# The first chunk of an RWKV, soft-MoE and FFN kernel: products with u moved between engines, and one load of expert weights asked for earlier

## Chip, core and metric

One core of one Trainium2 chip. The metric is the device time of one execution in microseconds (us); lower is better. A run of the kernel before is told by the median of three timed executions; one more execution was profiled.

## What is computed

Three stages in a row, all in fp32 at the interface. The first, an RWKV recurrence, is the one that the change touches:

```python
def _attn_ref(r, k, v, w, u):           # r, k, v: (4, 8, 768, 48); w, u: (8, 48)
    for t in range(S):
        kt, vt, rt = (k[:, :, t], v[:, :, t], r[:, :, t])
        cur = np.einsum('bhd,bhe->bhde', u[None] * kt, vt)
        y[:, :, t] = np.einsum('bhd,bhde->bhe', rt, state + cur)
        state = w[None, :, :, None] * state + np.einsum('bhd,bhe->bhde', kt, vt)
```

Its output, laid out as x of 3072 tokens by 384, goes through a soft mixture of 8 experts with 4 slots each: logits = x @ phi, a softmax over the tokens that gathers the slots' inputs, per expert relu(slot @ w1) @ w2, and a softmax over the slots that spreads the results. The last stage is h = x @ w_in (384 by 2048), g = h * sigmoid(1.702 h), g @ w_out.

## The kernel before

The recurrence is done in chunks of 128 time steps: 6 chunks (C) of 4 batches (B), so 24 steps (c, b), which this text numbers n = 4c + b, from batch 0 to batch 23. The work of one batch:

- VectorE scales r and k, which come as one transposed tile rkb, with powers of w (`scale`, L761, writes rks); TensorE multiplies them to scores (`scores`, L369); VectorE masks the scores (`mask`, L783, writes at).
- The term of the own time step, the bonus sum(r * k * u) * v. The product r*k is made by GpSimd from a second, untransposed tile krb (`bonus`, L1189, writes rkn), the product with u (ubc, u on all 128 partitions) by GpSimd, but in the first chunk by VectorE (L777). VectorE sums over the 48 channels of a head (`bonus_sum`, L770, writes dds). GpSimd multiplies v with the sums (`bonus_values`, L1209, writes vd). TensorE turns vd into the outputs' accumulators (`bonus_turns`, L388, line L396), in the first chunk one batch late, except for the chunk's last batch.
- TensorE adds the earlier state's part (`earlier`, L402) and scores times v (`outputs`, L419), ScalarE copies the result to yt (`columns`, L996).
- GpSimd makes scaled keys (`scaled_keys`, L1201, writes kk, with wkn, powers of w that TensorE turned and ScalarE copied), TensorE multiplies them with v (`state`, L430), VectorE adds that to the state (`new_state`, L798), which ScalarE first decays with four activations (`decay`, L1006).
- TensorE turns yt back (`tokens`, L441), ScalarE copies it (`rows`, L1014). From the second chunk on, the soft-MoE's running softmax over tokens runs with it.

Every engine runs its own program in the order of the code and waits on semaphores. TensorE's order for a batch is: earlier part of the batch before, scores of this batch, bonus turns (first chunk), outputs, state and token turns of batches before. The functions `step` of each engine set this order. The first chunk is written out, chunks 1 to 4 are a loop, the last chunk is written out.

SyncE (SP) issues the loads in one line: rkb, krb and v of a batch, with two buffers for rkb and krb. The load of rkb n waits until VectorE has scaled batch n-2, that of krb n until GpSimd has made the keys of n-2; each waits in the line, so what is behind it waits too. Behind each batch's loads from the second chunk on stand one or two pieces (512 KB each) of the expert weights w1 (`load_w1`, L283), 24 in all, four of them in the last chunk. ScalarE's queue loads the identity, u (128 copies), the mask, and, after it has copied wkn, phi in five small loads (L992, L994). At the start TensorE does dummy products (`keep_warm`, L361) until the first scores are possible: ten, and seven more after the first scores.

After the scan come the experts (L556 to L615) and the FFN (`tile`, L696), in which TensorE works through three fp32r products per 128x512 tile.

## Time and profile before

| | us |
|---|---|
| median of three timed executions | 389.01 |
| lowest and highest | 386.53, 389.36 |
| the profiled execution | 385.76 |
| its span in the trace | 383.8 |

The span runs from the first to the last recorded instruction; the profiled execution's own time is 1.96 us longer. A "batch" in the scan is a period of some 4.4 us. The times in all rows are counted from the span's start. In a row of the timeline the first number is the start, the second the time until the merged instructions have ended, and in brackets stands how long the engine was idle before and what ended that. fp32 products are issued in two passes, so that a row of eight products counts x16.

### The profile page before, as it was taken

To read this page: it belongs to the slowest core of one execution; us is meant where nothing else is said; L and a number is where in the kernel's file an instruction comes from. 1 tells how busy PE (TensorE), PEld (TensorE's weight loads), DVE (VectorE), ACT (ScalarE), POOL (GpSimd) and SP (SyncE) were. 2 spreads that over 40 slices of the span, in tenths; PEclk is the share of its full clock that TensorE was granted. 3 is DMA by queue.
4 is the path that set the end of the run, shared out by engine and by line. 5 is a ranking of instruction groups with operands and counts; after the bars stand their busy time and mean duration, and the time that the engine had idled before them with its cause. 6 is when DMAs were issued, how large, how long until landed. Compare 5 with 4: busy or idle time off the path is not lost.

```text
span 383.8 us, 9102 instructions
## 1 busy us (share of the span) xinstructions
PE 370.8 (97%) x3212; PEld 291.3 (76%) x3212; DVE 236.2 (62%) x433; ACT 189.4 (49%) x410; POOL 92.4 (24%) x109
## 2 busy tenths in 40 slices
PE   5699999999999999999999999999999999999996
PEld 5578787878877344568888888888888888888885
DVE  6988696978784201678756556555555555555550
ACT  1345454544435341676564456445644564465552
POOL 4777897888672100000000000000000000000000
PEclk9999999999999999999999999999999999999999
DMA  7899999999999899600011002000200020002002
GB/s 232 293 340 392 395 360 401 376 404 400 402 345 412 344 379 413 258 0 2 1 40 45 0 2 82 0 0 0 82 0 0 0 82 0 0 0 82 0 2 82
DMA packets 21797, 63.76 MB, mean 166 GB/s; under 512 B 3088, under 2 KB 6816, under 8 KB 21392
## 3 DMA queue, kind: packets, MB, share of 16 engines
q1 hardware_dynamic: 20864, 63.09, 43.3%
q10 hardware_dynamic: 912, 0.39, 0.6%
q8 instruction: 14, 0.23, 0.2%
q14 instruction: 7, 0.06, 0.0%
HBM read 58.75 MB, written 4.72 MB: 165 GB/s over the span
## 4 chain that ended last, share of the span: by engine, by line
PE 91%; DVE 3%; DMA 2%; issue 1%; ACT 1%; POOL 1%; SPq 0%; DVEq 0%; ACTq 0%
PE bank L639 11%; PE bank L637 11%; PE bank L638 11%; PE bank L377 6%; PE pair L425 6%; PE pair L637 6%; PE pair L638 5%; PE pair L639 5%; PE bank L622 4%; PE pair L413 3%; PE pair L396 3%; PE bank L584 3%; PE bank L446 3%; PE bank L564 2%; PE bank L437 2%; DMA vb<-v 2%
## 5 line engine op out<-in xcount | busy, mean ns | idle before, releaser
L921 DVE TENSOR_TENSOR gf<-bank,sg 128x512 f32<-128x512 f32 x72 | 49.7, 691 | 59.3 <-ACT sg L1119 58.9
L1119 ACT ACTIVATE sg<-bank 128x512 f32<-128x512 f32 x72 | 42.9, 598 | 73.4 <-PE bank L622 73.4
L637 PE MATMUL bank<-glo,whi 128*128 128x512 f32 x190 | 73.9, 389 | 0.0
L639 PE MATMUL bank<-ghi,wlo 128*128 128x512 f32 x190 | 73.9, 389 | 0.0
L638 PE MATMUL bank<-ghi,whi 128*128 128x512 f32 x190 | 73.9, 389 | 0.0
L927 DVE TENSOR_TENSOR glo<-gf,ghi 128x512 fp32r<-128x512 f32 x96 | 66.2, 690 | 1.0 <-ACT ghi L1125 0.7
L1125 ACT ACTIVATE ghi<-gf 128x512 fp32r<-128x512 f32 x96 | 60.0, 625 | 2.0 <-DVE gf L921 1.9
L639 PEld LDWEIGHTS bank<-ghi,wlo 128*128 128x128 f32 x190 | 35.7, 188 | 7.4
L637 PEld LDWEIGHTS bank<-glo,whi 128*128 128x128 f32 x190 | 35.7, 188 | 7.4
L638 PEld LDWEIGHTS bank<-ghi,whi 128*128 128x128 f32 x190 | 35.7, 188 | 7.4
L767 DVE TENSOR_TENSOR rks<-rkb,bank 112x512 f32<-112x512 f32 x48 | 30.7, 681 | 12.9 <-PE pair L413 6.6
L637 PE MATMUL pair<-glo,whi 128*128 128x512 f32 x95 | 37.2, 391 | 0.5 <-DVE glo L927 0.4
L638 PE MATMUL pair<-ghi,whi 128*128 128x512 f32 x95 | 37.0, 389 | 0.0
L639 PE MATMUL pair<-ghi,wlo 128*128 128x512 f32 x95 | 37.0, 389 | 0.0
L793 DVE COPY_PREDICATED at<-keep,bank 128x512 f32<-128x512 int32 x48 | 32.6, 731 | 1.3 <-PE bank L377 0.9
L377 PE MATMUL bank<-rks 48*128 48x128 f32 x384 | 27.9, 284 | 5.2 <-DVE rks L767 3.8
L377 PEld LDWEIGHTS bank<-rks 48*128 48x128 f32 x384 | 23.4, 187 | 9.5 <-issue 7.9
L921 DVE TENSOR_TENSOR gf<-pair,sg 128x512 f32<-128x512 f32 x24 | 16.6, 691 | 22.6 <-ACT sg L1119 22.5
L1002 ACT ACTIVATE yt<-pair 112x512 f32<-112x512 f32 x24 | 14.3, 597 | 29.3 <-PE pair L425 29.3
L622 PE MATMUL bank<-ct,mst 128*128 (+1 forms) x72 | 27.9, 392 | 0.4 <-DVE mst L951 0.4
L1194 POOL TENSOR_TENSOR rkn<-krb 128x384 f32<-128x384 f32 x24 | 24.1, 1003 | 12.1 <-DMA krb<-kr 11.7
L425 PE MATMUL pair<-at,vb 128*48 128x128 f32 x384 | 25.9, 277 | 0.0
(183 smaller groups left out, 512.6 us busy)
## 6 DMA issues: line engine op xcount, KB each, us to landing
ring<-w SPq DMA_DIRECT2D x24, 512.0 KB, 6.3
rkb<-rk SPq DMA_DIRECT2D x23, 512.0 KB, 6.0
krb<-kr SPq DMA_DIRECT2D x24, 384.0 KB, 5.7
ring<-w SPq DMA_DIRECT2D x4, 1536.0 KB, 13.8
ring<-w SPq DMA_DIRECT2D x8, 768.0 KB, 9.7
vb<-v SPq DMA_DIRECT2D x24, 192.0 KB, 5.6
out<-ob SPq DMA_DIRECT2D x18, 256.0 KB, 2.1
ring<-win SPq DMA_DIRECT2D x3, 1024.0 KB, 14.9
```

The lines of the kernel that those rows point to most:

```text
L377: last = pe.matmul(SC[i][:, hp * CH:(hp + 1) * CH], rks[s, b % 2, 1, hp, :], rks[s, b % 2, 0, hp, :], start=True, stop=True)
L425: last = pe.matmul(YT[i][o0:o0 + D, a * CH:(a + 1) * CH], vb[:, b, 2 * (a + 2 * w) + i, :], at[:, b % 2, i, a + 2 * w, :], start=False, st ...
L622: pe.matmul(HB[f % 4][:, :], mst[:, f * P:(f + 1) * P], ct_flat[:, bass.ds(i * TT, TT)], start=True, stop=True).then_inc(hh_ps, 1)
L637: pe.matmul(o, w_hi, lo, start=(f == 0), stop=False)
L638: pe.matmul(o, w_hi, hi, start=False, stop=False)
L639: pe.matmul(o, w_lo, hi, start=False, stop=(f == KF - 1)).then_inc(prod_ps, 1)
L767: dve.tensor_tensor(rks[a, b % 2, x, :, :], rkb[a, b % 2, x, :, :], w[a, :, :], ALU.mult)\
L793: dve.copy_predicated(at[:, b % 2, half, :, :], keep[:, :].unsqueeze(1).to_broadcast([P, 4, CH]), SC[half][:, :].rearrange("p (h t) -> p h ...
L921: dve.tensor_tensor(gf[:, f % 2, :], bank[f % 4][:, :], sg[:, f % 2, :], ALU.mult).then_inc(gf_ok, 1)
L927: dve.tensor_tensor(glo[:, f % 4, :], gf[:, f % 2, :], ghi[:, f % 4, :], ALU.subtract)\
L1119: act.activation(sg[:, f % 2, :], bank[f % 4][:, :], ACT.Sigmoid, scale=1.702).then_inc(sg_ok, 1)
L1125: act.activation(ghi[:, f % 4, :], gf[:, f % 2, :], ACT.Copy).then_inc(ghi_ok, 1)
```

## The change

It touches the first chunk (c = 0) and three orders.

- u is loaded to one partition; DVE sets 128 ones in a row of lnat, TensorE multiplies ones and u (a product over one row, 384 columns), ScalarE copies the result to all partitions of ubc. The dummy products are three ahead of it, six behind it (WARM) and eight after the first scores.
- In the first chunk GpSimd does the products with u, as in the others. Its `step` is split: the r*k product of batch 1 stands ahead of the scaled keys of batch 0.
- In the first chunk ScalarE makes vd from v, by eight activations of 48 columns with the sum as scale, one per head, ahead of `columns` of the batch before. It no longer decays the zero states of batches 0 to 2.
- VectorE scales batch n+1 ahead of mask of batch n for all n of the first chunk, and sums batch n between the two. The sum waits for the bonus turns of two batches back, no longer for vd alone.
- phi's five loads move from ScalarE's queue to SP, ahead of batch 2's loads.
- One piece of w1 is asked for behind batch 3's loads; every later piece moves up by one, and the last batch has none.

```diff
@@ -40,7 +40,7 @@
 LEAD = 3
-WARM = 10
+WARM = 6
@@ -190,6 +190,7 @@
             sem(n) for n in ("lt_ps", "l_ok", "cm_ok", "nm_ok", "ex_ok", "al_ok", "tr_ps", "tr_ok", "p_ps", "run_ok"))
+        s_u, ones_ok, u_ps, u_ok, vd_first = (sem(n) for n in ("s_u", "ones_ok", "u_ps", "u_ok", "vd_first"))
         nm_new, l_new, mask_go, tiles_go = (sem(n) for n in ("nm_new", "l_new", "mask_go", "tiles_go"))
@@ -297,16 +298,22 @@
             load_v(0, 1)
+            for o0, w in HEADS:
+                for p0, i in HEADS:
+                    sp.dma_start(phs[o0:o0 + D, :, :].rearrange("p (a i) s -> p a i s", i=2)[:, :, i, :],
+                                 phi[p0:p0 + D, 2 * w:2 * w + 2, :]).then_inc(s_phi, 16)
+            sp.dma_start(phs[D:64, :, :], phi[D:64, :, :]).then_inc(s_phi, 16)
             step(0, 2, 0, 0)
-            step(0, 3, 0, 0)
+            step(0, 3, 0, 1)
             for dst, src in ((same[:, :], match), (jcol[:, :], jsel), (pick[:, :, :], sel)):
...
                 for b in range(B):
-                    step(c, b, (B + 1) * (c - 1) + b, 1 if b < B - 1 else 2)
+                    step(c, b, (B + 1) * (c - 1) + 1 + b, 1 if b < B - 1 else 2)
             for b in range(B):
-                step(C - 1, b, (B + 1) * (C - 2) + b, 1)
+                step(C - 1, b, (B + 1) * (C - 2) + 1 + b, 1 if b < B - 1 else 0)
@@ -363,6 +370,12 @@
+            keep_warm(LG, 3)
+            pe.wait_ge(ones_ok, 1)
+            pe.wait_ge(s_u, 16)
+            pe.matmul(YN[:, 0:DM], lnat_flat[0:1, 0:P], ubc[0:1, :, :].rearrange("p h e -> p (h e)"),
+                      start=True, stop=True).then_inc(u_ps, 1)
             keep_warm(LG, WARM)
@@ -380,17 +393,18 @@
                     pe.wait_ge(wks_done, 1)
+                    pe.wait_ge(u_ok, 1)
                     for i in range(HP):
...
                     last.then_inc(wkn_ps, 1)
-                    keep_warm(LG, 7)
+                    keep_warm(LG, 8)
...
                 wait(pe, yt_ok, n)
-                wait(pe, vd_ok, n + 1)
+                wait(pe, *((vd_first, n + 1) if is_first(c) else (vd_ok, n - B + 1)))
                 for i in range(2):
@@ -721,6 +735,7 @@
+            dve.memset(lnat_flat[0:1, 0:P], 1.0).then_inc(ones_ok, 1)
             dve.memset(acc[:, :], 0.0).then_inc(run_ok, 1)
@@ -769,22 +784,15 @@
                 n = B * c + b
-                if is_first(c):
-                    dve.wait_ge(rk_ok, n + 1)
-                    if b == 0:
-                        dve.wait_ge(s_const, 16 * 2)
-                    dve.tensor_tensor(rkn[:, b % 2, :, :], rkn[:, b % 2, :, :], ubc[:, :, :], ALU.mult)\
-                       .then_inc(rku_ok, 1)
                 dve.wait_ge(rku_ok, n + 1)
-                wait(dve, vd_ok, n - 1)
+                wait(dve, vd_used, n - 1)
                 dve.tensor_reduce(dds[:, b % 2, :], rkn[:, b % 2, :, :], AX_X, ALU.add).then_inc(dd_ok, 1)
...
                     dve.wait_ge(zeroed, 5)
-                    dve.wait_ge(s_const, 16 * 2)
+                    dve.wait_ge(s_const, 16)
                 for half in range(2):
@@ -798,7 +806,11 @@
                 dve.wait_ge(st_ps, n + 1)
-                dve.wait_ge(sdec, HP * (n + 1))
+                if is_first(c):
+                    dve.wait_ge(s_new, 1)
+                else:
+                    dve.wait_ge(sdec, HP * (n - B + 2))
                 dve.tensor_tensor(st[a, b, :, :].rearrange("p h e -> p (h e)"),
@@ -843,16 +855,14 @@
                     slot_max(c - 1)
+                if more:
+                    scale(*following(c, b))
                 if is_first(c) and b:
-                    mask(c, b)
-                    scale(*following(c, b))
-                else:
-                    if more:
-                        scale(*following(c, b))
-                    mask(c, b)
+                    bonus_sum(c, b)
+                mask(c, b)
                 if is_last(c) and b == 2:
                     row_sum(*early)
-                if more:
+                if more and (tail or b == B - 1):
                     bonus_sum(*following(c, b))
@@ -979,19 +989,28 @@
             act.dma_start(idt[:, :], ident).then_inc(s_ident, 16)
-            for dst, src in ((ubc[:, :, :].rearrange("p h e -> p (h e)"), u.partition_broadcast(P)),
-                             (keep[:, :], strict)):
-                act.dma_start(dst, src).then_inc(s_const, 16)
+            act.dma_start(ubc[0:1, :, :].rearrange("p h e -> p (h e)"), u.partition_broadcast(1)).then_inc(s_u, 16)
+            act.dma_start(keep[:, :], strict).then_inc(s_const, 16)
+            act.wait_ge(u_ps, 1)
+            act.activation(ubc[:, :, :].rearrange("p h e -> p (h e)"), YN[:, 0:DM], ACT.Copy).then_inc(u_ok, 1)
...
                            ACT.Copy).then_inc(wkn_ok, 1)
-            for o0, w in HEADS:
-                for p0, i in HEADS:
-                    act.dma_start(phs[o0:o0 + D, :, :].rearrange("p (a i) s -> p a i s", i=2)[:, :, i, :],
-                                  phi[p0:p0 + D, 2 * w:2 * w + 2, :]).then_inc(s_phi, 16)
-            act.dma_start(phs[D:64, :, :], phi[D:64, :, :]).then_inc(s_phi, 16)
+            def bonus_values(c, b):
+                n = B * c + b
+                act.wait_ge(dd_ok, n + 1)
+                act.wait_ge(v_in[b], 16)
+                wait(act, vd_used, n - 1)
+                if b == 0:
+                    act.wait_ge(zeroed, 5)
+                for w in range(2):
+                    for x in range(HP):
+                        h = HP * w + x
+                        last = act.activation(vd[:, b % 2, x, w, 0:D], vb[:, b, h, :], ACT.Copy,
+                                              scale=dds[:, b % 2, h:h + 1])
+                last.then_inc(vd_first, 1)
@@ -1042,12 +1061,14 @@
                 tail = not is_first(c)
+                if not tail:
+                    bonus_values(c, b)
                 if tail and b == 1:
...
                 if not is_first(c, b):
-                    if not is_last(prev(c, b)[0]):
+                    if not is_first(prev(c, b)[0]) and not is_last(prev(c, b)[0]):
                         decay(*prev(c, b))
@@ -1186,16 +1207,20 @@
-            def bonus(c, b):
+            def products(c, b):
                 n = B * c + b
...
                     .then_inc(rk_ok, 1)
-                if is_first(c):
-                    return
+            def factors(c, b):
+                n = B * c + b
+                s = b % 2
                 pool.wait_ge(rk_ok, n + 1)
+                if is_first(c, b):
+                    pool.wait_ge(u_ok, 1)
                 pool.tensor_tensor(rkn[:, s, :, :], rkn[:, s, :, :], ubc[:, :, :], ALU.mult).then_inc(rku_ok, 1)
@@ -1211,8 +1236,6 @@
                 wait(pool, vd_used, n - 1)
-                if is_first(c, b):
-                    pool.wait_ge(zeroed, 5)
                 pool.tensor_tensor(vd[:, b % 2, :, :, 0:D].rearrange("p x w e -> p w x e"),
@@ -1220,15 +1243,17 @@
             def step(c, b):
+                products(c, b)
                 if b == 1 and is_first(c):
                     scaled_keys(0, 0)
-                bonus(c, b)
+                factors(c, b)
                 if not is_last(c) and not is_first(c, b):
...
                     pool.tensor_tensor(*row_terms(1, 0, EARLY), ALU.mult).then_inc(c_ok, 1)
-                bonus_values(c, b)
+                if not is_first(c):
+                    bonus_values(c, b)
                 if is_last(c) and b == 1:
```

The places on which the prediction rests, as each engine's program has them. First VectorE from the state's sum of batch 0 to the end of the first chunk, before (rks is scaled, dds are the sums, at the masked scores, st the state):

```order
L802 TENSOR_TENSOR st<-st,bank 112x192
L793 COPY_PREDICATED at<-keep,bank 128x512 x2
L767 TENSOR_TENSOR rks<-rkb,bank 112x512 x2
L777 TENSOR_TENSOR rkn<-rkn,ubc 128x384
L781 TENSOR_REDUCE dds<-rkn 128x8
L802 TENSOR_TENSOR st<-st,bank 112x192
L793 COPY_PREDICATED at<-keep,bank 128x512 x2
L767 TENSOR_TENSOR rks<-rkb,bank 112x512 x2
L781 TENSOR_REDUCE dds<-rkn 128x8
L802 TENSOR_TENSOR st<-st,bank 112x192
```

and with the change:

```order
L814 TENSOR_TENSOR st<-st,bank 112x192
L782 TENSOR_TENSOR rks<-rkb,bank 112x512 x2
L789 TENSOR_REDUCE dds<-rkn 128x8
L801 COPY_PREDICATED at<-keep,bank 128x512 x2
L814 TENSOR_TENSOR st<-st,bank 112x192
L782 TENSOR_TENSOR rks<-rkb,bank 112x512 x2
L789 TENSOR_REDUCE dds<-rkn 128x8
L801 COPY_PREDICATED at<-keep,bank 128x512 x2
L789 TENSOR_REDUCE dds<-rkn 128x8
L814 TENSOR_TENSOR st<-st,bank 112x192
```

The products with u are gone, and both dds rows (batch 2, 3) stand behind the scaling of the next batch and ahead of the mask of their own. ScalarE from its first copy to the end of the first chunk, before:

```order
L987 ACTIVATE wkn<-bank 128x384
L992 DMA phs<-phi 48x2x32 x4
L994 DMA phs<-phi 16x128
L1011 ACTIVATE st<-st,pw 112x48 x4
L1002 ACTIVATE yt<-pair 112x2x2x128
L1011 ACTIVATE st<-st,pw 112x48 x4
L1002 ACTIVATE yt<-pair 112x2x2x128
L1019 ACTIVATE yn<-bank 128x384
L1011 ACTIVATE st<-st,pw 112x48 x4
L1002 ACTIVATE yt<-pair 112x2x2x128
L1019 ACTIVATE yn<-bank 128x384
```

and with the change (x16 is batches 0 and 1):

```order
L995 ACTIVATE ubc<-bank 128x384
L998 ACTIVATE wkn<-bank 128x384
L1011 ACTIVATE vd<-vb,dds 128x48 x16
L1021 ACTIVATE yt<-pair 112x2x2x128
L1011 ACTIVATE vd<-vb,dds 128x48 x8
L1021 ACTIVATE yt<-pair 112x2x2x128
L1038 ACTIVATE yn<-bank 128x384
L1011 ACTIVATE vd<-vb,dds 128x48 x8
L1021 ACTIVATE yt<-pair 112x2x2x128
L1038 ACTIVATE yn<-bank 128x384
```

The decays (st) are gone, and each batch's eight vd activations stand ahead of the copy (yt) of the batch before. SP's line from the end of batch 1's loads on, before:

```order
L268 DMA rkb<-rk 128x1024
L276 DMA krb<-kr 128x768
L281 DMA vb<-v 128x384
L268 DMA rkb<-rk 128x1024
L276 DMA krb<-kr 128x768
L281 DMA vb<-v 128x384
L304 DMA same<-match 128x128
L304 DMA jcol<-jsel 128x4
L304 DMA pick<-sel 128x64
```

and with the change:

```order
L304 DMA phs<-phi 48x2x32 x4
L306 DMA phs<-phi 16x128
L269 DMA rkb<-rk 128x1024
L277 DMA krb<-kr 128x768
L282 DMA vb<-v 128x384
L269 DMA rkb<-rk 128x1024
L277 DMA krb<-kr 128x768
L282 DMA vb<-v 128x384
L286 DMA ring<-w 128x1024
L311 DMA same<-match 128x128
L311 DMA jcol<-jsel 128x4
L311 DMA pick<-sel 128x64
```

phi stands ahead of batch 2's loads, one weights piece behind batch 3's and ahead of the three constants; the loads of batch 4 follow in the loop.

## Rows read from the trace of the kernel before

**Rows 1.** The page: engine totals, and the chain that ended last.
```profile
PE 370.8 (97%) x3212; PEld 291.3 (76%) x3212; DVE 236.2 (62%) x433; ACT 189.4 (49%) x410; POOL 92.4 (24%) x109
...
PE 91%; DVE 3%; DMA 2%; issue 1%; ACT 1%; POOL 1%; SPq 0%; DVEq 0%; ACTq 0%
```

**Rows 2.** Timeline of TensorE in the first chunk.
```profile
2.81 4.00 PE L364 MATMUL bank<-idt 128*128 128x128 f32 x20 [2.81 <-DMA idt<-ident]
...
17.56 1.16 PE L377 MATMUL bank<-rks 48*128 48x128 f32 x16 [1.74 <-DVE rks L767]
...
22.00 1.16 PE L377 MATMUL bank<-rks 48*128 48x128 f32 x16 [0.79 <-DVE rks L767]
...
25.48 0.62 PE L396 MATMUL pair<-idt,vd 128*112 128x128 f32 x4
...
26.61 1.16 PE L377 MATMUL bank<-rks 48*128 48x128 f32 x16
```

**Rows 3.** VectorE: groups of 0 to 22 us (busy, mean ns, idle); then its timeline.
```profile
L777 DVE TENSOR_TENSOR rkn<-rkn,ubc 128x384 f32<-128x384 f32 x4 | 3.3, 833 | 1.0 <-POOL rkn L1194 1.0
...
13.07 1.33 DVE L777 TENSOR_TENSOR rkn<-rkn,ubc 128x384 f32<-128x384 f32 x1 [0.41 <-POOL rkn L1194]
...
18.27 0.55 DVE L781 TENSOR_REDUCE dds<-rkn 128x8 f32<-128x384 f32 x1
...
19.32 1.37 DVE L793 COPY_PREDICATED at<-keep,bank 128x512 f32<-128x512 int32 x2 [0.24 <-issue]
20.58 1.27 DVE L767 TENSOR_TENSOR rks<-rkb,bank 112x512 f32<-112x512 f32 x2
```

**Rows 4.** Timelines of GpSimd (POOL) and ScalarE (ACT), first chunk.
```profile
11.08 1.00 POOL L1206 TENSOR_TENSOR kk<-krb,wkn 128x384 f32<-128x384 f32 x1
...
18.90 0.83 POOL L1216 TENSOR_TENSOR vd<-vb,dds 128x384 f32<-128x384 f32 x1 [1.08 <-DVE dds L781]
...
12.27 1.01 ACT L1011 ACTIVATE st<-st,pw 112x48 f32<-112x48 f32 x4 [1.99 <-issue]
...
20.36 0.60 ACT L1002 ACTIVATE yt<-pair 112x512 f32<-112x512 f32 x1 [3.36 <-PE pair L425]
```

**Rows 5.** Windows: busy time by engine, TensorE's granted clock, DMA share, GB/s.
```profile
4.80:5.30 0.50, 0.50 (x4) 0.50 (x4) 0.37 (x4) 0.00 (x0) 0.00 (x0) 1.00 1.02 158
12.00:16.00 4.00, 3.11 (x52) 2.69 (x52) 3.55 (x6) 1.50 (x5) 2.92 (x5) 1.00 0.77 234
16.00:20.00 4.00, 2.44 (x34) 2.17 (x36) 3.72 (x8) 1.00 (x5) 2.92 (x4) 1.00 0.92 301
32.00:36.00 4.00, 4.00 (x66) 3.46 (x69) 3.46 (x7) 3.12 (x12) 3.11 (x5) 1.00 1.04 409
```

**Rows 6.** Timeline of SP: start and duration of the issue of each load.
```profile
3.21 0.59 SPq L276 DMA_DIRECT2D krb<-kr  x1
...
12.11 0.33 SPq L276 DMA_DIRECT2D krb<-kr  x1
...
12.96 0.43 SPq L268 DMA_DIRECT2D rkb<-rk  x1
...
14.39 0.43 SPq L281 DMA_DIRECT2D vb<-v  x1
...
17.61 0.35 SPq L268 DMA_DIRECT2D rkb<-rk  x1
```

**Rows 7.** Issue to landing (us), of those at 3.21, 12.96, 14.39, 17.61.
```profile
krb<-kr SPq DMA_DIRECT2D x1, 384.0 KB, 7.6
...
rkb<-rk SPq DMA_DIRECT2D x1, 512.0 KB, 5.2
...
vb<-v SPq DMA_DIRECT2D x1, 192.0 KB, 5.3
...
rkb<-rk SPq DMA_DIRECT2D x1, 512.0 KB, 4.6
```

## The prediction

> **What bounds the kernel now.** I read the page's engine totals and its chain first, to see which engine the end of the span hangs on: TensorE is busy for 370.8 of 383.8 us and holds 91% of the chain [rows 1]. So what TensorE does not lose in a gap is not to be won. Then TensorE's own timeline, for where its gaps are: in the first chunk it waits up to 1.74 us before a batch's scores, last before the fourth batch's at 22.00, and from there it runs on: turns of the fourth bonus at 25.48, scores of the fifth batch at 26.61 [rows 2]. Everything behind 25.48 is a stretch that follows TensorE. The change is therefore worth what it moves the instant 25.48, the turns of the fourth batch's bonus values (L396); I call it T.
>
> What holds TensorE up to 22.00 is VectorE, which is nearly without gaps there: scaling of a batch's r and k 1.27 us, masks 1.37 us, and a product of r*k with u that takes 3.3 us over four, one of them 1.33 us, with GpSimd at work beside it [rows 3]. The transfers come third: from 12 to 20 us the 16 DMA engines carry 234 and 301 GB/s at a busy share of 0.77 and 0.92, against 409 GB/s in the stretch where the expert weights run with them [rows 5]. They are busy with slow packets, not waiting for work. Nothing waits for them in the kernel before at this place, because VectorE is later.
>
> **The change part by part.** Batches are numbered 0 to 3 in the first chunk, 4 is the first of the second.
>
> *Start.* The load of u to 128 partitions (192 KB) becomes a row of one partition, a TensorE product with ones and a ScalarE copy. While the 192 KB run, the DMA engines carry 158 GB/s at a share of 1.02 [rows 5]. 192 KB at 409 GB/s is 0.5 us, and some 1.5 us at 158 instead of 409 GB/s lose 0.9 more: the loads behind it land up to 1.4 us earlier. The second batch's k,r pair, issued at 3.21 and 7.6 us on its way [rows 6, 7], lands at 9.4 instead of 10.8; the low end of this term is 0.5 (the bytes alone), giving 10.3. Ten dummy products took 4.0 us from 2.81 on [rows 2]; now three, a ones product of 384 columns (as three of them) and six more are twelve, 4.8 us, to 7.6. The first scores start there instead of at 8.06, and u lies ready long before GpSimd wants it. The transposed wkn is ready near 9.9.
>
> *GpSimd.* Its three products are 1.00 us each [rows 4]. It now does r*k of batch 1 ahead of the keys of batch 0, so these keys end at 9.4 + 1.0 + 1.0 = 11.4 (before: 12.08). The load of batch 2's k,r pair waits for them: 11.5 instead of 12.11 [rows 6]. That is the whole gain of the queue, 0.6 us: the loads behind it stand in one line on SP.
>
> *VectorE.* Its four products with u go (3.3 us), GpSimd does them 1.0 us each, beside it. GpSimd has batch 1's product with u at 12.4, VectorE scales batch 2 to 13.2 (its load is there by 12), sums to 13.6, masks batch 1 to 14.9: scores of batch 2 start there instead of at 17.56. But the order turns round: the r,k scaling of batch n+1 now stands ahead of the sum and the mask of batch n. In the kernel before the scaling of 3 began at 20.58 and that of 4 after the mask of 3, when their loads had long landed. Now they ask early, and the load is what is late.
>
> *The loads.* Load of r,k for batch 3: issued 12.96, 5.2 us on its way, so at 18.16, which is 6.05 us behind the issue at 12.11 [rows 6, 7]. With that issue at 11.5 it lands at 17.55. Scaling 3 then runs to 18.8, sum 0.55, mask of 2 to 20.6; scores of 3 start at 20.65, 1.35 ahead of 22.00. The v load of batch 3 (14.39 + 5.3 = 19.7, so 1.5 behind the r,k load) comes at 19.1. Behind it now stands the piece of expert weights: 524 KB at 409 GB/s, 1.3 us, to 20.4. Then three small constants and the r,k load of batch 4. Before, it landed at 17.61 + 4.6 = 22.2, 2.5 us behind v though it had been in the queue for 2 us by then [rows 6, 7]. At full rate its own bytes are 1.3 us. Some of the slow start may now lie under the weights, so I take the middle, 1.9: it lands at 22.3, within 21.7 to 22.9. The removed 0.6 and the weights' 1.3 and 0.6 of cover cancel: no earlier than before.
>
> *From there to T.* Scaling of 4: 22.4 to 23.65. Sum of batch 3: to 24.15 (VectorE, 0.55 us, behind the scaling in its order). ScalarE: eight activations of 128x48. The trace has four of 112x48 in 1.01 us at 323 ns for one [rows 4], a spacing of 0.23, so 0.32 + 7 x 0.23 = 1.93; before, GpSimd did this in one of 0.83. Behind them on ScalarE, in order, stands the copy of batch 2's outputs (0.60), for which the turns of batch 3 wait too. With 0.1 of hand-over: 24.15 + 0.1 + 1.93 + 0.60 = 26.8. T moves from 25.48 to 26.8: 1.3 us later. TensorE's other work is no cover: from 20.65 its own row of work (25.48 - 22.00 = 3.5 us) would bring it there at 24.1.
>
> *At nothing:* the 16 decays of zero states that ScalarE no longer does in the first chunk (it waited 3.36 us for TensorE at 20.36 anyway [rows 4]); the wait of the sums for the turns of two batches back (done by 16.7 for batch 3); fewer dummy products. The first weights piece leaves the end of the fifth chunk's loads: no wait of TensorE for weights stands in the chain there (DMA has 2% of it, [rows 1]); worth 0 to -0.2.
>
> Sum: profiled 385.76 us (span 383.8 and 1.96 around it) + 1.3 = 387.1. The three other runs have a median of 389.01, 3.25 above the profiled one; there 390.3.
>
> Bounds of T. All loads from the first byte after 11.5 on at 409 GB/s: 2.85 MB in 7.0 us land batch 4's r,k at about 20; then T is set by scores of 3 and T gains 1.35, at most 2.2 if batch 3's load gains as well. If u's load cost only its bytes and the k,r pair still comes at 10.3: keys at 12.3, line 0.9 later than forecast, T at 27.7; with the end term at 2.5, 28.3, 2.8 late.
>
> The small loads. Phi's five loads of 8 to 12 KB move from ScalarE's queue into SP's line ahead of batch 2's r,k. At 12 to 16 us, where most of them finished before, the share was only 0.77 [rows 5], so the trace gives them little weight: I count 0.5 us, and batch 2's load still lands by 12. The Trainium skill, DMA: Bandwidth & Descriptors, Rules for kernel authors, says that transfers under 64 KB are mostly overhead, and its measured table has 0.68 us for a 4 KB one. By that, as an estimate, five would put 3.4 us ahead of the line. The same page says that queues of different issuing engines end on the same 16 DMA engines, which speaks for no change. The 5.2 us above, in which this line ran slowly without them, leaves both open.
>
> **Rivals.**
> A, the forecast: the r,k load of batch 4 and the scaling in front of the sum set T; 1.3 later, 390.3.
> B, faster: VectorE was the only bound. It holds if batch 4's r,k lands before 21.0 (T = landing + 4.5 then meets 25.48). For it: the share of 0.92 at 301 GB/s [rows 5] leaves a faster line possible with more in flight. Against: the slow packets. Gain 1.35 from scores of 3 at 20.65: 387.7.
> C, no change: landing near 21.0, T within 0.3 of before: 389.0.
> D, slower by much: TensorE now has two gaps of about 2.0 and 2.7 us (before 20.65 and before 26.8), before at most 1.74, after which sixteen score products took 1.16 us as everywhere [rows 2]. If its clock falls to 1.2 GHz in one, a batch of 4.4 us (22.00 to 26.61 less a gap) takes up to twice that: 3.2 on top of A, 393.5. The Trainium skill, TensorE: Matmul & The Clock Gate, HAM oscillation, describes this for kernels that wait for transfers; no row of this case shows it. The same size comes if the small loads cost 3 us.
>
> **How the numbers follow.** A 0.52, B 0.25, C 0.13, D 0.10. A alone spans 389.2 to 391.8. The range takes in most of B below, and the spread of the runs shown (386.5 to 389.4), and a part of D: 387.0 to 392.4. 1% is 3.9 us, about what a measurement of this kernel tells from no change. Faster by more (below 385.1) needs B with double its gain: 0.03. Slower by more is D's upper half: 0.06. The rest is within 1%.
>
> **What would show it.** Right: r,k scaling of batch 4 waits for its load, which lands at 21.7 to 22.9; eight activations in about 1.9 us; the fourth turns wait for ScalarE and start at 26.2 to 27.5; behind them the timeline is the old one, shifted. Keys of batch 0 at 11.4, scores of 3 near 20.65. Wrong: the scaling of 4 finds its data there and the turns start before 25.4 (B); sixteen score products longer than 1.2 us (D); new gaps of TensorE after 30 us, which this working excludes.

## The result and the profile after

The changed kernel takes 389.70 us (median of 20 executions, 386.06 to 391.34), the kernel before, run beside it, 386.41 us (20 executions, 385.29 to 389.97). The ratio is 1.007, with a 95% interval of 1.0051 to 1.0088: slower, by 2.7 us. (The medians are 3.3 apart; after's executions fall into two groups, of which more below, and its median lies in the upper one.) The three executions of before that were shown ahead of the prediction, with their median of 389.01, are among these 20 and lay high.

The profiled execution of after took 390.45 us, with a span of 388.7 against 383.8. The page: engine totals, TensorE's granted clock in 40 slices of the span, and the chain's shares.

```profile
PE 376.6 (97%) x3214; PEld 296.1 (76%) x3214; DVE 234.2 (60%) x430; ACT 194.0 (50%) x431; POOL 93.4 (24%) x109
...
PEclk9986999999999999999999999999999999999999
...
PE 89%; DMA 3%; ACT 2%; SPq 1%; DVE 1%; issue 1%; POOL 1%; DVEq 0%; ACTq 0%; POOLq 0%
```

Against [rows 1], VectorE has lost 2.0 us of work and ScalarE has gained 4.6. TensorE is busy for 5.8 us more with two instructions more: its work has grown longer, not larger. The third and fourth clock digits (8 and 6, from 19 to 39 us) say where. In the chain, TensorE and VectorE have two percent less each; DMA, ScalarE and the SP queue have one more each. TensorE's timeline in the first chunk:

```profile
8.80 1.39 PE L390 MATMUL bank<-rks 48*128 48x128 f32 x16
...
15.49 1.16 PE L390 MATMUL bank<-rks 48*128 48x128 f32 x16
...
21.69 1.16 PE L390 MATMUL bank<-rks 48*128 48x128 f32 x16 [2.55 <-DVE at L801]
22.87 1.05 PE L410 MATMUL pair<-idt,vd 128*112 128x128 f32 x4
...
28.81 0.65 PE L410 MATMUL pair<-idt,vd 128*112 128x128 f32 x4 [1.84 <-ACT yt L1021]
...
30.09 2.08 PE L390 MATMUL bank<-rks 48*128 48x128 f32 x16
```

These answer to [rows 2]. Batch 2's scores start 2.07 us earlier than before (15.49 for 17.56), batch 3's only 0.31 (21.69 for 22.00), and T, the turns of batch 3's bonus values, comes at 28.81 instead of 25.48, after a wait of 1.84 for ScalarE. From 22.9 on, products take up to twice as long, with a pause around 27 to 29 us: the four turns 1.05 instead of 0.65, batch 4's sixteen score products 2.08 instead of 1.16. The windows of after (busy time of PE, PEld, DVE, ACT, POOL, then granted clock, DMA share, GB/s) have the granted clock at 0.50, the lower of TensorE's two levels, in two stretches, some 23 to 27 and 30 to 37 us:

```profile
22.00:24.00 2.00, 1.98 (x22) 1.45 (x20) 0.00 (x0) 1.19 (x4) 0.74 (x1) 0.74 1.02 396
24.00:26.00 2.00, 2.00 (x28) 1.94 (x30) 1.42 (x3) 0.00 (x0) 0.29 (x1) 0.50 1.04 409
...
30.00:32.00 2.00, 2.00 (x20) 1.78 (x16) 1.29 (x2) 1.01 (x4) 1.69 (x2) 0.50 0.93 318
34.00:36.00 2.00, 2.00 (x25) 1.91 (x22) 0.53 (x2) 0.93 (x2) 1.22 (x2) 0.50 0.71 289
```

VectorE, to be read against [rows 3]: its scalings now wait for transfers, and the sum of batch 3 stands behind the second of them.

```profile
18.64 1.29 DVE L782 TENSOR_TENSOR rks<-rkb,bank 112x512 f32<-112x512 f32 x2 [2.68 <-DMA rkb<-rk]
...
24.58 1.28 DVE L782 TENSOR_TENSOR rks<-rkb,bank 112x512 f32<-112x512 f32 x2 [2.72 <-DMA rkb<-rk]
25.78 0.55 DVE L789 TENSOR_REDUCE dds<-rkn 128x8 f32<-128x384 f32 x1
```

ScalarE and GpSimd, against [rows 4]: the copy of wkn, for which GpSimd's first keys wait, and in front of T the eight activations with the copy of batch 2's outputs behind them.

```profile
10.76 0.49 ACT L998 ACTIVATE wkn<-bank 128x384 f32<-128x384 f32 x1 [4.22 <-PE bank L398]
...
26.36 1.91 ACT L1011 ACTIVATE vd<-vb,dds 128x48 f32<-128x48 f32 x8 [3.18 <-DVE dds L789]
28.18 0.57 ACT L1021 ACTIVATE yt<-pair 112x512 f32<-112x512 f32 x1
...
11.33 1.00 POOL L1231 TENSOR_TENSOR kk<-krb,wkn 128x384 f32<-128x384 f32 x1 [1.04 <-ACT wkn L998]
```

SP's line, against [rows 6]: the first load behind GpSimd's keys of batch 0, the weights piece, and the r,k load of batch 4.

```profile
12.36 0.35 SPq L277 DMA_DIRECT2D krb<-kr  x1
...
15.12 0.44 SPq L286 DMA_DIRECT2D ring<-w  x1
...
17.82 0.35 SPq L269 DMA_DIRECT2D rkb<-rk  x1
```

And how long the last two of these were on their way (last number), against [rows 7]:

```profile
ring<-w SPq DMA_DIRECT2D x1, 512.0 KB, 7.9
...
rkb<-rk SPq DMA_DIRECT2D x1, 512.0 KB, 6.7
```

The whole path to T stands in these rows: load issued at 17.82, landed at 24.5, scaling, sum to 26.3, activations to 28.3, copy to 28.75, turns. The same load took 4.6 us before, issued at 17.61 [rows 7], and nobody waited for it.

How the distance between the two profiled executions grows along the program, by the start of a batch's scores:

| | before | after | later by |
|---|---|---|---|
| T | 25.48 | 28.81 | 3.33 |
| scores of batch 4 | 26.61 | 30.09 | 3.48 |
| scores of batch 9 | 50.70 | 56.34 | 5.64 |
| first expert product | 127.28 | 132.15 | 4.87 |

So 3.3 us had been lost by T, 2.2 more in the stretch at low clock behind it, and 0.8 came back by the experts.

### The profile page after: what moved, and what is told of

The parts are those of the page before. It is cut to its first block, busy times and chain, and to the rows that moved or that the text cites. A ratio compares the mean times of both kernels' runs of the same rounds, so it can differ in the third digit from the quotient of the medians.

```text
span 388.7 us, 9123 instructions
## 1 busy us (share of the span) xinstructions
PE 376.6 (97%) x3214; PEld 296.1 (76%) x3214; DVE 234.2 (60%) x430; ACT 194.0 (50%) x431; POOL 93.4 (24%) x109
## 4 chain that ended last, share of the span: by engine, by line
PE 89%; DMA 3%; ACT 2%; SPq 1%; DVE 1%; issue 1%; POOL 1%; DVEq 0%; ACTq 0%; POOLq 0%
PE bank L653 11%; PE bank L651 11%; PE bank L652 11%; PE bank L390 6%; PE pair L439 6%; PE pair L651 5%; PE pair L653 5%; PE pair L652 5%; PE bank L636 4%; PE pair L427 3%; PE bank L598 3%; PE pair L410 3%; PE bank L460 3%; PE bank L578 2%; DMA rkb<-rk 2%; PE bank L451 2%
## 5 line engine op out<-in xcount | busy, mean ns | idle before, releaser
L390 PE MATMUL bank<-rks 48*128 48x128 f32 x384 | 29.0, 292 | 2.6 <-DVE at L801 2.6
L390 PEld LDWEIGHTS bank<-rks 48*128 48x128 f32 x384 | 24.3, 194 | 7.0 <-issue 4.0
L439 PE MATMUL pair<-at,vb 128*48 128x128 f32 x384 | 27.7, 289 | 0.0
```

The lines of the kernel that those rows point to most:

```text
L390: last = pe.matmul(SC[i][:, hp * CH:(hp + 1) * CH], rks[s, b % 2, 1, hp, :], rks[s, b % 2, 0, hp, :], start=True, stop=True)
L439: last = pe.matmul(YT[i][o0:o0 + D, a * CH:(a + 1) * CH], vb[:, b, 2 * (a + 2 * w) + i, :], at[:, b % 2, i, a + 2 * w, :], start=False, st ...
```

## The experiments

Ten kernels were run, each beside the kernel before. "Line" is the time from the first SP issue behind the keys of batch 0 (12.36 in after) to the landing of batch 4's r,k load, or to the scaling that waited for it. Before has 12.11 and some 10.1 us.

### One part taken out of the change

**The weights piece, back at the fifth chunk's end.**

```diff
-            step(0, 3, 0, 1)
+            step(0, 3, 0, 0)
```

(and the later pieces' numbers with it). Expected: 

> The changed kernel, with the piece of expert weights back at the end of the scan (none behind batch 3's loads). Theory L (the landing of batch 4's r,k load sets the turns of batch 3, at 28.81 us in the changed kernel): the load lands 1.3 us earlier (512 KB at about 400 GB/s), near 23.2 instead of 24.5, the turns start near 27.4, and the time falls by 1.3 to 2 us, to about 388 where the changed kernel has 389.7. Rival V (VectorE's and ScalarE's own work sets the turns, whatever the load does): turns within 0.3 us of 28.8, time unchanged. Rival P (the piece helps at the end of the scan): time rises by the 1.3 us that it saved there.

Measured: 386.70 us, ratio 1.0033 [1.0001, 1.0065]. Timeline of VectorE, then of TensorE:

```profile
23.48 1.28 DVE L782 TENSOR_TENSOR rks<-rkb,bank 112x512 f32<-112x512 f32 x2
24.69 0.54 DVE L789 TENSOR_REDUCE dds<-rkn 128x8 f32<-128x384 f32 x1
...
27.71 0.65 PE L410 MATMUL pair<-idt,vd 128*112 128x128 f32 x4 [0.60 <-ACT yt L1021]
...
28.88 1.16 PE L390 MATMUL bank<-rks 48*128 48x128 f32 x16
```

The line had begun at 13.44, 1.1 later than in after (wkn was late here, 11.85), and still the load was there at 23.4: 10.0 us behind its head, as before, where after needs 12.2. So theory L holds (the load at 23.4 for 23.2, T at 27.71 for 27.4), and rivals V and P do not. The clock stayed up. The piece costs some 2 us of the line: in the twelve profiles of this document the line takes 11.2 to 12.2 us with it (six) and 9.4 to 10.3 without (six). By the ratios, half of the loss goes with it (0.33% left of 0.70%), but the interval is wide. The mean clock was 0.99 in only 3 of 11 executions, which took 389.9 to 390.8 us; the other eight have a median of 386.15, which is before's (386.08). The time fell by more than expected because most executions also kept their clock.

**Sum and mask ahead of the scaling.**

```diff
+                ahead = is_first(c) and b
-                if more:
+                if more and not ahead:
                     scale(*following(c, b))
-                if is_first(c) and b:
+                if ahead:
                     bonus_sum(c, b)
                 mask(c, b)
+                if more and ahead:
+                    scale(*following(c, b))
```

Expected: 

> The changed kernel, with VectorE's order in batches 1 to 3 turned: sum, mask, and only then the scaling of the next batch, so that neither sum nor mask stands behind a load. Theory L: sum of batch 3 near 21.9 instead of 25.78, the turns of batch 3 near 25.0 instead of 28.8, scores of batch 4 near 26 (behind the scaling, its load lands near 24.5 still). TensorE's second gap is under 1 us, its clock stays full (sixteen score products 1.16 us). Time 3.5 to 5 us under the changed kernel, 384.5 to 386 and so at or a little under the kernel before. Rival V (ScalarE's eight activations and GpSimd's products are the cause): turns not before 27.5, time at most 1.5 us under the changed kernel.

Measured: 386.46 us, ratio 1.0017 [0.9998, 1.0035]; one execution of 2068.53 us, left out of the ratio, has no explanation here. Timeline of VectorE, then of TensorE:

```profile
22.99 0.54 DVE L789 TENSOR_REDUCE dds<-rkn 128x8 f32<-128x384 f32 x1
24.26 1.36 DVE L801 COPY_PREDICATED at<-keep,bank 128x512 f32<-128x512 int32 x2 [0.72 <-PE bank L390]
25.50 1.27 DVE L782 TENSOR_TENSOR rks<-rkb,bank 112x512 f32<-112x512 f32 x2
...
26.43 0.62 PE L410 MATMUL pair<-idt,vd 128*112 128x128 f32 x4
```

The weights piece is still in the line here, and the load lands at 25.0. But the sum of batch 3 no longer stands behind the scaling of batch 4: it comes at 22.99 (after: 25.78), and T at 26.43 without a wait. The order alone gives back three quarters of the loss (0.17% left of 0.70%); whether that is more than the piece alone gives (386.46 and 386.70 us) is inside the spread. The time is 0.5 above the expected range. T is 1.4 above the value expected since batch 3's scores start at 22.96: the first products ran slow again (2.08 us for sixteen) and wkn was late.

**phi's loads back on ScalarE's queue, behind the copy of wkn.**

```diff
-                    sp.dma_start(phs[o0:o0 + D, :, :].rearrange(...
+                    act.dma_start(phs[o0:o0 + D, :, :].rearrange(...
```

Expected: 

> The changed kernel, with phi's five small loads back on ScalarE's queue behind its copy of wkn. Theory L gives them no part: batch 2's r,k load (landed 11.4, used 11.68) lands 0.5 us earlier for nothing, the loads of batch 2 to 4 land within 0.3 us of before, the vd activations of batch 0 come up to 2.3 us later on ScalarE for nothing, time within 0.7 us of 389.7. Rival S (small transfers ahead of the line slow it): batch 4's r,k load lands over 1 us earlier and the time falls by that.

Measured: 389.98 us, ratio 1.0085 [1.0052, 1.0118], the same as after; T at 28.76. Where the five small loads stand plays no part. This profile shows one thing more: the gap ahead of batch 3's scores is 0.98 us here (after: 2.55), the clock stays up until 29.9, and T and the first expert product (132.08) still come as in after (28.81 and 132.15). So the first of after's two stretches at low clock cost nothing, since T waited for the load anyway; the price lies in the second. The Trainium skill, DMA: Bandwidth & Descriptors, Rules for kernel authors, calls transfers below 64 KB mostly overhead, and the estimate from it was 3.4 us in this line; no such time shows in either position.

**The bonus values of the first chunk by GpSimd, as before.**

```diff
-                wait(pe, *((vd_first, n + 1) if is_first(c) else (vd_ok, n - B + 1)))
+                wait(pe, vd_ok, n + 1)
...
-                if not tail:
-                    bonus_values(c, b)
...
-                if not is_first(c):
-                    bonus_values(c, b)
+                bonus_values(c, b)
```

Expected: 

> The changed kernel, with the bonus values of the first chunk made by GpSimd in one product of 0.83 us, as before the change, instead of ScalarE's eight activations of 1.91 us. Theory L, its ScalarE term: the sum of batch 3 still ends near 26.3, its values are ready near 27.3, the copy of batch 2's outputs on ScalarE no longer stands behind them; turns of batch 3 near 27.3 instead of 28.8, time 1.5 us lower, more where the clock then does not fall. Rival: GpSimd's products of the next batches are put off by 0.83 us each and the turns stay near 28.8.

Measured: 388.08 us, ratio 1.0055 [1.0029, 1.008]. Timeline of VectorE, then of TensorE:

```profile
24.91 0.55 DVE L789 TENSOR_REDUCE dds<-rkn 128x8 f32<-128x384 f32 x1
...
28.42 0.55 DVE L789 TENSOR_REDUCE dds<-rkn 128x8 f32<-128x384 f32 x1 [1.72 <-POOL rkn L1222]
...
21.42 1.16 PE L390 MATMUL bank<-rks 48*128 48x128 f32 x16 [2.14 <-DVE at L801]
...
23.09 1.75 PE L439 MATMUL pair<-at,vb 128*48 128x128 f32 x16
...
26.50 0.74 PE L410 MATMUL pair<-idt,vd 128*112 128x128 f32 x4
```

From the sum to T it is 1.6 us (24.91 to 26.50); after has 3.0 (25.78 to 28.81). So the eight activations and the copy behind them cost 1.4 us. (The clock fell here too: sixteen output products took 1.75 us, 1.08 at full clock, and the granted clock is 0.50 from 24 to 26 us.) But GpSimd, which does the bonus values ahead of the next batch's products, now is late in turn: the next sum waits 1.72 us for its product. From 1.1 us at batch 4's scores (27.76) the kernel falls 1.9 behind by batch 9's (52.6). T is 0.8 earlier than expected, far from the rival's 28.8, but what the rival said of GpSimd's next products came true one batch later. By the ratios (0.55% and 0.70%, intervals that overlap) the kernel is not told apart from after.

### The clock

**Dummy products in the two gaps**, ten ahead of batch 3's scores and eight ahead of its turns.

```diff
+                if is_first(c) and b == 3:
+                    keep_warm(LG, 10)
                 wait(pe, masked, 2 * n)
...
+                if is_first(c) and b == 3:
+                    keep_warm(LG, 8)
```

Expected: 

> The changed kernel, with ten dummy products of TensorE ahead of its wait for the fourth batch's scores and eight ahead of its wait for the fourth batch's turns, to fill the gaps of 2.55 and 1.84 us; nothing else. Theory C (of the 4.9 us, some 3.3 are the late turns and 1.5 to 2.5 the clock that fell to half between 23 and 37 us): turns still near 28.8, sixteen score products of batch 4 in 1.16 us instead of 2.08, granted clock 1.00 throughout, time 1.5 to 2.5 us under the changed kernel, near 387.7. Rival (the clock cost nothing, since something else bounded TensorE there): time unchanged.

Measured: 387.83 us, ratio 1.0043 [1.0026, 1.006]. Two windows, and TensorE's timeline:

```profile
30.00:32.00 2.00, 2.00 (x36) 1.58 (x34) 0.82 (x2) 0.93 (x5) 1.60 (x3) 1.00 0.92 349
34.00:36.00 2.00, 2.00 (x53) 1.52 (x52) 0.74 (x4) 0.49 (x1) 2.00 (x3) 1.00 0.96 375
```

```profile
29.80 0.65 PE L414 MATMUL pair<-idt,vd 128*112 128x128 f32 x4 [0.56 <-ACT yt L1025]
...
30.97 1.16 PE L392 MATMUL bank<-rks 48*128 48x128 f32 x16
```

T is later than in after by 1.0, but not for the dummies: it waits 0.56 us for ScalarE. The first scores took 2.08 us here, wkn came late (11.88), and the line started at 13.47 instead of 12.36. Still the kernel is faster: by 1.9 us in the medians, by 1.0 in the ratios (whose intervals just touch, 1.0026 to 1.006 and 1.0051 to 1.0088). So the clock's share is of that size. All its six executions had a mean clock of 0.999 or 1.000. (This mean does not see the start: the granted clock reads 1.00 from 8 to 10 us, where sixteen score products take 2.08 us. There only durations tell.) After splits in the same way: the 7 of its 20 executions at 0.996 or above have a median of 387.81, the 13 below one of 390.42. 13 of 20 times the 2.6 us between them is 1.7, which agrees with the dummies' gain. So the same program meets it in some executions and not in others, and with this change in most; the kernel before had 0.991 or less in 8 of the 81 executions that ran beside the ten kernels. The Trainium skill, TensorE: Matmul & The Clock Gate, HAM oscillation, describes such a loss for a kernel whose products wait 3 to 5 us for transfers. The trace agrees in kind, but here the waits are 2.55 and 1.84 us long, and for VectorE and ScalarE, which stood behind a transfer.

**The ones product behind nine dummy products instead of three.**

```diff
-WARM = 6
+WARM = 0
...
-            keep_warm(LG, 3)
+            keep_warm(LG, 9)
```

Expected: 

> The changed kernel, with TensorE's ones product behind nine dummy products instead of behind three (none after it): the same products in another order. Theory G (the 1.6 us in which one row of TensorE works for the ones product keep its clock from rising, so the first scores still run low): the clock is up at the first scores (sixteen products in 1.16 us, not 1.39 or 2.08), the copy of wkn ends about 1 us earlier, keys of batch 0 and all loads behind them with it, turns of batch 3 near 27.5 to 28, time 1 us under the changed kernel. Rival: the time of the rise is chance and has nothing to do with the ones product: scores of batch 0 at 1.39 to 2.08 us as before, time unchanged.

Measured: 388.82 us, ratio 1.0058 [1.0037, 1.0079]. Its timeline of TensorE:

```profile
7.98 1.16 PE L390 MATMUL bank<-rks 48*128 48x128 f32 x16
...
27.32 0.67 PE L410 MATMUL pair<-idt,vd 128*112 128x128 f32 x4 [3.47 <-ACT yt L1021]
...
28.95 2.08 PE L390 MATMUL bank<-rks 48*128 48x128 f32 x16
```

With the first scores at full clock the copy of wkn comes at 9.71, SP's line starts at 11.67 and T follows at 27.32, near what was expected. But the wait ahead of T is now 3.47 us, and the clock falls behind it; the mean clock is 0.989 to 0.991 in each of the twelve executions. The time is 0.9 us under after's, with ratio intervals that overlap. Whether the order of the products sets the clock's first rise is not shown: the same order in a later kernel (below, the fastest) had its sixteen first score products at 2.08 us.

### What is left when both causes go

**Sum and mask first, and no early weights piece**: the first two edits together. Expected: 

> Sum and mask ahead of the scaling on VectorE, and the weights piece back at the end of the scan. Theory L: with the sum freed from the load, the earlier landing of batch 4's r,k is worth little at the turns of batch 3 (26.43 in the run with only the order turned); it gives chunk 1 an earlier batch 5 (landing 29.1 there, scaling started 29.23). If TensorE's gap near 33 us was that, it goes: 385.0 to 386.0, under the run with only the order turned (386.5). Rival: the order alone had all of it: 386.5.

Measured: 386.83 us, ratio 1.0013 [0.9987, 1.0039]. T came at 25.30, the first expert product at 126.84 (before: 25.48 and 127.28). With both causes out, the loss is gone, and so is the hoped-for gain: the time is 0.8 above the expected range, near the rival's 386.5. The timelines of GpSimd, VectorE and TensorE show what sets T in their place:

```profile
20.16 1.00 POOL L1218 TENSOR_TENSOR rkn<-krb 128x384 f32<-128x384 f32 x1 [1.19 <-DMA krb<-kr]
...
22.26 0.55 DVE L789 TENSOR_REDUCE dds<-rkn 128x8 f32<-128x384 f32 x1 [0.98 <-POOL rkn L1227]
...
25.30 0.65 PE L410 MATMUL pair<-idt,vd 128*112 128x128 f32 x4 [0.49 <-ACT yt L1024]
```

The product with u, 3.3 us less on VectorE, is now what VectorE waits for. And the path begins at a load once more: batch 3's k,r load lands at 20.05, then come GpSimd's r*k product, its product with u, the sum, the eight activations and the copy. In the kernel before, the same load was there at 19.1 and GpSimd took it up at 19.68 without a wait.

**The same with the ones product late** as well. Expected: 

> As the run above, and the ones product behind nine dummy products. If theory G holds, the first scores run at full clock, the keys of batch 0 end near 11.3 instead of 12.4 to 13.4, and the turns of batch 3 start near 25: at or before the kernel before's 25.48. Time 384.5 to 385.5, under the kernel before (386.1). If G does not hold: as the run above.

Measured: 385.65 us, ratio 0.9965 [0.994, 0.999]: the only kernel of the study that is faster than the one before, by 1.4 us, and all its executions had a mean clock of 0.996 or more. TensorE's timeline, then ScalarE's:

```profile
8.52 2.08 PE L390 MATMUL bank<-rks 48*128 48x128 f32 x16
...
26.25 0.62 PE L410 MATMUL pair<-idt,vd 128*112 128x128 f32 x4
...
25.57 0.60 ACT L1024 ACTIVATE yt<-pair 112x512 f32<-112x512 f32 x1 [0.27 <-PE pair L439]
```

The copy now waits for TensorE, not TensorE for the copy. But the expected start did not come in this profiled execution: the first scores took 2.08 us, T came at 26.25 for an expected 25, and the first expert product at 127.52, later than in the kernel before (127.28). So why the median is lower is not shown; the gain over the kernel without the late ones product (386.83) is not told apart from the spread.

### The start

**The kernel before, with only u made by the ones product.** Expected: 

> The kernel before, with one part of the change: u loaded to one partition, multiplied with ones on TensorE behind three dummy products (six behind it) and copied by ScalarE. All orders are those of the kernel before. Theory K (the earlier landing of the first loads is not worth anything by itself, since the keys of batch 0 wait for wkn, which the slow first scores make late): batch 1's k,r lands near 9.2 instead of 10.8, but wkn is copied at 10.8 or later instead of 9.79, keys of batch 0 end at 12.3 or later (before 12.08), turns of batch 3 within 0.7 us of 25.48, time 386 to 387. Rival (the 1.4 us of the loads carry through): turns near 24.3, time 385.0 or less.

Measured: 386.77 us, ratio 1.0009 [0.9996, 1.0022]. Batch 1's k,r load (issued at 3.10) from issue to landing, then TensorE's timeline:

```profile
krb<-kr SPq DMA_DIRECT2D x1, 384.0 KB, 6.7
```

```profile
17.84 1.16 PE L384 MATMUL bank<-rks 48*128 48x128 f32 x16 [2.46 <-DVE rks L776]
...
19.51 1.87 PE L433 MATMUL pair<-at,vb 128*48 128x128 f32 x16
```

The load lands at 9.8 instead of 10.8, but the line starts at 12.40, not earlier than before (12.11), because wkn (10.80) is later than the load. By itself the new start is worth nothing. And behind a wait of 2.46 us the clock is down in this profile (19.6 to 23 us), with none of the change's other edits; T came at 26.44, 0.3 beyond the expected 0.7 from 25.48.

**The kernel without both causes, but with u loaded to 128 partitions and ten dummy products as before.** Expected: 

> Sum and mask ahead of the scaling, the weights piece back at the end, and u loaded to 128 partitions as in the kernel before, with ten dummy products and no ones product. Theory K: TensorE's clock is up by the first scores (16 in 1.16 us at 8.1), wkn is ready at 10.3, batch 1's k,r lands at 10.8, keys of batch 0 end at 12.8, near what the run with the ones product has; the turns of batch 3 start between 25.3 and 26.3, time 385.3 to 386.3, like the best run (385.65) within 0.5. Rival (the cheap u is what makes the best run good): 387 or more.

Measured: 386.45 us, ratio 0.9996 [0.9979, 1.0013], not told apart from 386.83, and between the theory's 385.3 to 386.3 and the rival's 387; T came at 25.37, as expected. Here wkn is early (9.63) and the load late, 7.7 us on its way to 10.9; the keys of batch 0 start at 11.88. Of the two things that the keys wait for, each way of making u moves one forward and the other back.

## Why the prediction was right, and where it was not

The forecast was 390.3 us, 1.3 above 389.01; measured are 389.70, but with a base of 386.41. That the absolute time was met is luck: the base was 2.6 too high, and the move was forecast as 0.3% and is 0.7%. The side and the mechanism of A hold, and rival D, which had 0.10, came true on top of it in most executions. Of the signs named for A, the wait of the scaling for the load, the eight activations and the wait of the turns for ScalarE came; the landing (24.5 for at most 22.9), T (28.81 for at most 27.5, and past the latest bound of the working, 28.3) and the old timeline behind T did not.

**The mechanism.** "The r,k load of batch 4 and the scaling in front of the sum set T" is what the chain and the bracket `[2.72 <-DMA rkb<-rk]` show, and each of its two halves was taken out alone: without the piece 386.70, with the sum first 386.46, with both 386.83 against 386.39 of before in that comparison. The last part, eight activations ahead of the copy, was sized right (1.91 for a predicted 1.93) and costs 1.4 us in the run with GpSimd.

**Keys of batch 0 at 11.4: wrong, 12.33.** The load was early, as predicted (landed at 9.2 for 9.4). The step that failed was the one by which the first scores start at 7.6 and wkn is ready near 9.9. They started at 8.80 and took 1.39. The twelve products' worth ahead of them took 6.0 us (2.79 to 8.80), not 4.8. The 0.4 for each came from the ten of before [rows 2], which ran partly at the upper level; here all ran at the lower, 0.5 for a dummy and 1.64 for the ones product. wkn was there at 11.25, and the line started at 12.36 instead of 11.5. The run with the ones product late had a fast start and 11.67: the rest of that step was sound.

**Landing of batch 4's r,k at 22.3: wrong, 24.5.** Of the 2.2 us, 0.9 is that late start and 0.3 lies in v of batch 3 (20.25 for 19.1). The rest, 1.1, lies between v and the r,k load, with the weights piece between them: 4.3 us for a predicted 1.3 + 1.9 = 3.2. How the 4.3 divides is not fixed: in after the piece landed 2.8 behind v and the load 1.5 behind the piece, in the run with phi's loads moved back 1.3 and 3.0. The size of the piece's term was the error. Against the 2.5 us from v to the load in before [rows 7], the working let it add 0.7 (1.3 of bytes, less 0.6 of cover); the six profiles with the piece have 3.2 to 4.9 us there, the six without it 1.6 to 2.5, some 2 us less in the mean.

**Scores of batch 3 at 20.65: 21.69**, 1.0 late for the same start (its load landed at 18.6, predicted 17.55). **T at 26.8: 28.81.** From landing to T, 4.3 us were measured and 4.5 predicted; the whole miss lies ahead of it.

**The clock.** Behind "two gaps of about 2.0 and 2.7 us" the clock was given a chance of one in ten to fall. The gaps were 2.55 and 1.84, and the mean clock was 0.991 or lower in 13 of 20 executions (0.996 or more in the other seven). In the profiled one, batch 4's scores to the experts then took 102.1 us, in the run with dummy products 99.7. The price in D, 3.2, was of the right size for an execution that meets it (2.6 between the two groups); the chance was the error.

**At nothing.** That held for phi's loads; the decays and the wait of the sums were not tried alone, and no row has a wait for them. Not foreseen was the path that is left when both causes are out: batch 3's k,r load, GpSimd's two products, the sum and the eight activations, with which T comes no earlier than before (25.30 for 25.48).

**A bound of the working.** The line at full rate was to land batch 4's r,k at about 20, but 2.85 MB in 7.0 us from 11.5 on end at 18.5. Nothing hung on it, as the load came at 24.5.

Two things stay open. That the change is worth what it moves T holds only in part. The kernels that are late at T take less time from there to the experts: 99.2 us from batch 4's scores without the piece and 99.7 with dummies, 100.7 before. Of the 2.2 us that T is late without the piece, 0.8 is left at the first expert product. So it is chance, too, that after's seven executions with the higher mean clock lie 1.4 us above before, near the forecast 1.3: T had moved by 3.3 in the profiled one. Which wait of the loop gives that back was not tried. And what sets the clock's first rise was not found.

## What to carry to other kernels

An engine that works in order should not have work that is ready behind work that asks for a load: putting the sum and the mask first again took away some three quarters of this loss with no transfer moved. A prefetch in the same queue ahead of loads that are waited for costs more than its bytes at full rate, here 2 us for the 1.3 of its bytes; put it where nothing behind it is urgent, even if it is not needed until later. And when a change opens gaps of some 2 us on TensorE, price the clock's fall as a likely case (here it came behind each of seven such waits), and look for it in the durations of one repeated instruction on both sides of the gap.

## Unexpected of the hardware

- In the twelve profiles, TensorE's granted clock fell to 0.50 within 2 us behind each of the seven waits of the scan that were longest: 1.79, 1.84, 2.14, 2.46, 2.55, 3.27 and 3.47 us. It stayed up behind 1.74 in before [rows 2] and behind the shorter ones, but once: in the run with the sum first it is down from some 35 us on, behind 1.27. So the length of one wait is not all of it. At low clock a row of sixteen score products takes 2.08 us for 1.16.
- The time of the clock's first rise varies between executions with the same instructions at the start. Three dummies, the ones product and six more gave first scores in 1.39 to 2.08 us. Nine dummies ahead of the ones product gave 1.16 us (at 7.98) in one kernel and 2.08 (at 8.52) in another; the copy of wkn followed, 9.71 and 11.57, and with it the start of SP's line, 11.67 and 13.17.
- A 192 KB load of one row to 128 partitions delays its neighbours by more than its bytes, which are 0.5 us at 409 GB/s: without it batch 1's k,r load was 5.8 to 7.0 us on its way in ten profiles, with it 7.6 and 7.7 in two.
